# Row sums turned on TensorE, every unit of the probabilities split, values without zero columns: one change to an attention and MLP kernel

## What is computed

```python
q_rot, k_rot = (rotate(q), rotate(k))
scores = scale * np.matmul(q_rot, k_rot.transpose(0, 1, 3, 2))
scores = scores - np.max(scores, axis=-1, keepdims=True)
attn = np.exp(scores)
attn = attn / (np.sum(attn, axis=-1, keepdims=True) + 1e-09)
x = np.matmul(attn, v)                    # heads side by side: (4, 576, 512)
xk, xr = mu_k * x + (1 - mu_k) * x_prev, mu_r * x + (1 - mu_r) * x_prev
x = 1 / (1 + np.exp(-(xr @ w_r))) * (np.maximum(xk @ w_k, 0) ** 2 @ w_v)
u = x + (np.maximum(x.transpose(0, 2, 1) @ w_tok1, 0) @ w_tok2).transpose(0, 2, 1)
out = u + np.maximum(u @ w_ch1, 0) @ w_ch2
```

## Time and profile before

| | us |
|---|---|
| median of 3 runs (1092.89 to 1094.23) | 1093.23 |
| the profiled execution, device time | 1097.79 |
| its span, first to last instruction | 1095.7 |
| attention slots, from the first slot that weighs to the last | 26.4 to 433.8 |

### The profile page before, as it was taken

How to read it: one execution, slowest core, us unless ns; L and a number is a source line. 1 busy time by engine, 2 the same in 40 slices (tenths; PEclk the granted TensorE clock), 3 DMA queues, 4 the chain that set the end, 5 groups by cost and what they waited for, 6 DMA issues and landing times.

```text
span 1095.7 us, 21136 instructions
## 1 busy us (share of the span) xinstructions
PE 997.6 (91%) x6976; PEld 942.4 (86%) x6976; DVE 634.7 (58%) x1232; ACT 533.6 (49%) x1280; POOL 298.3 (27%) x291
## 2 busy tenths in 40 slices
PE   4977977787798797999999999999999999999997
PEld 4876866676687686999999999888999999999997
DVE  5977876786788797886778766456312212212220
ACT  4976866676787687454444434353211211221220
POOL 6656555555476654300000000135000000000000
PEclk9988988988989999999999999999999999999999
DMA  4223322222322221300000000031000000000000
GB/s 97 59 57 71 71 60 49 58 55 61 69 54 50 44 37 24 97 14 0 0 0 0 0 0 0 1 115 58 1 22 1 22 22 0 22 22 0 22 22 22
DMA packets 93629, 37.70 MB, mean 34 GB/s; under 512 B 84000, under 2 KB 84896, under 8 KB 93600
## 3 DMA queue, kind: packets, MB, share of 16 engines
q1 hardware_dynamic: 93312, 37.00, 14.8%
q10 hardware_dynamic: 288, 0.33, 0.1%
HBM read 32.51 MB, written 4.80 MB: 34 GB/s over the span
## 4 chain that ended last, share of the span: by engine, by line
PE 57%; DMA 22%; SPq 8%; issue 7%; DVE 3%; ACT 2%; POOL 1%; POOLq 0%; DVEq 0%; ACTq 0%
DMA sum_rows<-rsums 19%; PE psum L635 18%; PE psum L637 18%; PE psum L636 18%; SPq L363 3%; SPq L362 3%; SPq L384 1%; DMA raw_qk<-in_k_dram 1%; DMA raw_v<-in_v_dram 1%; PE psum L723 1%; PE psum L799 1%; PE psum L588 1%; DVE k_lo L1173 1%; ACT stage_out L998 0%; SPq L368 0%
## 5 line engine op out<-in xcount | busy, mean ns | idle before, releaser
L588 PE MATMUL psum<-kT_hi,qT 128*128 128x288 f32 x320 | 113.9, 369 | 53.6 <-ACT probs L837 48.9
L1003 ACT ACTIVATE h_hi<-psum 128x288 fp32r<-128x288 f32 x96 | 39.4, 410 | 245.9 <-PE psum L637 245.9
L606 PE MATMUL psum<-ident,probs 128*128 128x128 f32 x800 | 131.5, 292 | 8.1 <-DVE pT_lo L1071 3.8
L1054 DVE TENSOR_REDUCE neg_max<-psum 128x1 f32<-128x576 f32 (+1 forms) x160 | 120.5, 753 | 6.5 <-PE psum L588 4.0
L606 PEld LDWEIGHTS psum<-ident,probs 128*128 128x128 f32 x800 | 99.0, 149 | 28.2 <-DVE pT_lo L1071 17.6
L588 PEld LDWEIGHTS psum<-kT_hi,qT 128*128 128x128 f32 x320 | 67.2, 210 | 63.9 <-ACT probs L837 49.4
L837 ACT ACTIVATE probs<-psum,neg_max 128x576 f32<-128x576 f32 (+1 forms) x160 | 118.4, 740 | 5.8 <-DVE neg_max L1054 3.3
L1245 DVE SCALAR_TENSOR_TENSOR h_lo<-psum,h_hi 128x288 fp32r<-128x288 f32 x96 | 43.9, 458 | 125.8 <-ACT h_hi L1003 125.8
L635 PE MATMUL psum<-u_hi,wc_hi 128*128 128x288 f32 x384 | 114.2, 297 | 0.2 <-DVEq L1239 0.2
L635 PE MATMUL psum<-h_hi,wc_hi 128*128 128x288 f32 x384 | 113.7, 296 | 0.0
L636 PE MATMUL psum<-u_lo,wc_hi 128*128 128x288 f32 x384 | 113.3, 295 | 0.0
(11 more groups left out here) (127 smaller groups left out, 2786.0 us busy)
## 6 DMA issues: line engine op xcount, KB each, us to landing
stage_w<-in_moe_w_ch_dram SPq DMA_DIRECT2D x8, 768.0 KB, 4.4
rb<-sum_rows SPq DMA_DIRECT2D x32, 144.0 KB, 4.4
out_dram<-stage_out SPq DMA_DIRECT2D x8, 576.0 KB, 3.7
raw_qk<-in_q_dram SPq DMA_DIRECT2D x32, 128.0 KB
raw_qk<-in_k_dram SPq DMA_DIRECT2D x32, 128.0 KB
raw_v<-in_v_dram SPq DMA_DIRECT2D x32, 128.0 KB
w_raw<-in_moe_w_k_dram SPq DMA_DIRECT2D x4, 512.0 KB, 5.9
w_raw<-in_moe_w_v_dram SPq DMA_DIRECT2D x4, 512.0 KB, 5.6
```

The source lines that it names most:

```text
L588: ins = t.matmul(bank[:, x, 0:HALF], qT[i][:, tile * P:(tile + 1) * P], keys[:, x * HALF:(x + 1) * HALF], start=(n == 0), stop=(n == 1))
L606: ins = t.transpose(bank[:, at:at + P], probs[i][:, tile, at_key:at_key + P], ident[:, :])
L1003: a.activation(h2_hi[:, f, :], psum[:, f % 4, 0:HALF], ACT.Relu).then_inc(h2_hi_ready, 1)
L1054: d_.tensor_reduce(neg_max[0:m, at:at + 1], score_banks[at][0:m, :, 0:HALF], AX.XY, ALU.max, negate=True).then_inc(maxed, 1)
```

## The change

- `WHOLE` is empty. Unit 0 is split as the others are: DVE gets L0 (128x512), and V0 becomes four matmuls on `v_pair`. `raw_v` loses its zero columns.
- The exponents' sums go into columns 64 to 68 of a 128x128 tile, one tile for each head of a pair. After unit 2 of the first span PE transposes that tile behind the 256 columns of `o_bank`; ACT's copy O0 becomes 448 wide and brings the turned sums along; DVE inverts rows of 128 on 5 partitions; SP stores them as five rows of 512 bytes.
- `invert` moves from the start of DVE's slot to its end, behind M4 and ahead of O1, and now waits for O0 of ACT.
- The store and the read of the sums move in SP's list. For the even head the read comes a store and several loads later. For the odd one store and read stand together.
- The three orders change; the last slot's too.
- `k2_hi` and `k2_lo` begin lower, over the end of `stage_w`, so SP waits for the end of `gated` before it loads the channel weights.

```diff
-    WHOLE = (0,)
+    WHOLE = ()
...
-    ORDER = steps("T0 T1 S0 P0 S1 T2 V0 T3 V1 V2 T4 S2 T5 P1 S3 V3 T6 T7 S4 V4 V5 V6 V7")
-    ACT_ORDER = steps("H0 H1 P0 P1 P2 H2 E0 H3 v0 O0 E1 H4 H5 E2 H6 H7 P3 E3 O1 E4")
-    DVE_ORDER = steps("I0 M0 L1 P0 P1 L2 M1 L3 P2 O0 M2 L4 L5 M3 L6 L7 M4 P3 O1")
+    ORDER = steps("S0 T0 T1 P0 S1 T2 V0 T3 V1 T4 S2 V2 T5 P1 S3 T6 V3 V5 T7 V4 S4 V6 V7")
+    ACT_ORDER = steps("H0 H1 E0 P0 H2 P1 P2 H3 E1 v0 H4 O0 H5 P3 E2 H6 H7 E3 O1 E4")
+    DVE_ORDER = steps("M0 L0 L1 M1 L2 P0 P1 L3 P2 M2 L4 O0 L5 M3 P3 L6 L7 M4 I0 O1")
...
-    LAST_DVE_ORDER = steps("I0 L0 L1 X0 L2 X1 L3 O0 X2 L4 X3 L5 X4 L6 X5 L7 X6 O1 X7")
+    LAST_DVE_ORDER = steps("L0 L1 X0 L2 X1 L3 O0 I0 X2 L4 X3 L5 X4 L6 X5 L7 X6 O1 X7")
...
-        raw_v = [r(f"raw_v{i}", [P, NT, P]) for i in range(2)]
-        o_lo = r("o_lo", [P, SPAN[1][2]])
+        raw_v = [r(f"raw_v{i}", [P, NT, D]) for i in range(2)]
+
+        SUMS = SPAN[1][2]
+        o_lo = r("o_lo", [P, SUMS + P])
...
-        sums = r("sums", [P, 2, NT])
-        rsums = r("rsums", [P, 2, NT])
+        sums = r("sums", [P, 2, P])
+        inverted = r("inverted", [P, P])
...
-        r = Region(STAGE_END, RB)
+        r = Region(STAGE_END - (STAGE - KT * S) * FLOAT, RB)
...
-                sp.dma_start(sum_rows[bass.ds(it * 2 + kk, 1), :].rearrange("o (t p) -> p (o t)", p=P),
-                             rsums[:, kk % 2, :], allow_slow_non_contiguous=True).then_inc(sums_stored, 16)
+                at = kk % 2 * D
+                sp.dma_start(sum_rows[bass.ds(it * 2 + kk, 1), :].rearrange("o (t p) -> t (o p)", p=P),
+                             inverted[at:at + NT, :]).then_inc(sums_stored, 16)
...
                 if not start:
-                    sums_out(it, -1)
+                    sums_back(it, -2)
                     next_v(it, 0)
-                    sums_back(it, -1)
...
-                sums_out(it, 0)
+                if not start:
+                    sums_out(it, -1)
+                    sums_back(it, -1)
                 next_v(it, 1)
-                sums_back(it, 0, first=start)
                 if more:
                     next_qk(it, 1)
+                sums_out(it, 0)
...
+            sp.wait_ge(v_ready, KD * CHUNKS)
             with sp.Fori(0, B) as b:
...
-                if n == WHOLE[-1]:
+                if n == 0:
                     ins.then_inc(v_used, 1)
+                if keys[-1] == FULL and s == 0:
+                    pe.wait_ge(expd, upto(it, kk, NT, NT))
+                    ins = t.transpose(o_bank[:, SUMS:SUMS + P], sums[:, i, :], ident[:, :])
...
-                             accum_out=sums[0:m, i, tile:tile + 1]).then_inc(expd, 1)
+                             accum_out=sums[0:m, i, D + tile:D + tile + 1]).then_inc(expd, 1)
...
-                width = SPAN[s][2]
+                width = SUMS + P if s == 0 else SPAN[s][2]
...
-                dve.wait_ge(expd, upto(it, kk, NT, NT))
+                me = slice(i * D, i * D + NT)
+                dve.wait_ge(o_lo_ready, upto(it, kk, 2, 1))
...
-                d_.tensor_scalar(rsums[:, i, :], sums[:, i, :], 1e-9, None, ALU.add).then_inc(sum_plus, 1)
+                d_.tensor_scalar(inverted[me, :], o_lo[me, SUMS:SUMS + P], 1e-9, None, ALU.add).then_inc(sum_plus, 1)
```

More of the change, by code:

```diff
@@ L163, in attention_rwkv_mixer @@
         sin = r("sin", [P, NT, D])
-        RB = (END - S * FLOAT - 160) // 32 * 32
+        RB = (END - S * FLOAT - 32 - 3 * P * FLOAT) // 32 * 32
         assert r.at - base <= RB
@@ L382, in sums_back @@
                 if i == 0 and not first:
-                    sp.wait_ge(x_scaled, it)
+                    sp.wait_ge(x_scaled, it + (kk // 2 + 1))
                 sp.dma_start(rb[i * D:i * D + D, :], sum_rows[bass.ds(it * 2 + kk, 1), 0:S].to_broadcast([D, S])).then_inc(rb_in, 16)
@@ L432, in _ @@
             last = HEADS // 2 - 1
+            sums_back(last, -2)
+            next_v(last, 0)
             sums_out(last, -1)
-            next_v(last, 0)
             sums_back(last, -1)
[L436 to L439, removed]
+            for kk in range(2):
+                sums_out(last, kk)
+                sums_back(last, kk)
             sp.wait_ge(span_out, 2 * HEADS)
@@ L510, in _ @@
             pool.sem_inc(k_roped, 1)
+            pool.sem_inc(x_scaled, 1)
             pool.wait_ge(tables_in, 32)
@@ L888, in slot @@
                             act.wait_ge(omu_ready, 1)
-                            act.wait_ge(x_scaled, KD)
+                            act.wait_ge(x_scaled, KD + 1)
                         mix2(0, 0, n, after=False)
@@ L933, in gated @@
                 if more:
-                    act.wait_ge(x_scaled, HEADS // 2)
+                    act.wait_ge(x_scaled, HEADS // 2 + 1)
                     for m in range(2 * KD):
@@ L1073, in invert @@
             def invert(it, i, kk, first):
-                dve.wait_ge(expd, upto(it, kk, NT, NT))
+                me = slice(i * D, i * D + NT)
+                dve.wait_ge(o_lo_ready, upto(it, kk, 2, 1))
                 if not first:
                     dve.wait_ge(sums_stored, it * 32 + (16 * kk - 16))
-                d_.tensor_scalar(rsums[:, i, :], sums[:, i, :], 1e-9, None, ALU.add).then_inc(sum_plus, 1)
+                d_.tensor_scalar(inverted[me, :], o_lo[me, SUMS:SUMS + P], 1e-9, None, ALU.add).then_inc(sum_plus, 1)
                 dve.wait_ge(sum_plus, upto(it, kk, 1, 1))
-                d_.reciprocal(rsums[:, i, :], rsums[:, i, :]).then_inc(sum_inv, 1)
+                d_.reciprocal(inverted[me, :], inverted[me, :]).then_inc(sum_inv, 1)
             def write_x(it, i, kk, s):
@@ L1114, in slot @@
                             wait_for_room(dve)
-                            dve.wait_ge(x_scaled, KD)
+                            dve.wait_ge(x_scaled, KD + 1)
                         mix(0, 0, n)
@@ L1129, in _ @@
             d_.memset(sums[:, :, :], 1.0)
+            d_.memset(o_bank[:, SPAN[0][2]:SUMS], 0.0)
             for i in range(2):
@@ L1133, in _ @@
                     d_.memset(raw_qk[i][TAIL:P, j, FULL, :], 0.0)
-                d_.memset(raw_v[i][:, :, D:P], 0.0)
                 d_.memset(rot_q[i][:, NT, :], 0.0)
@@ L1180, in gated @@
                 if more:
-                    dve.wait_ge(x_scaled, HEADS // 2)
+                    dve.wait_ge(x_scaled, HEADS // 2 + 1)
                     for m in range(2 * KD):
```

## The result

| | before | changed |
|---|---|---|
| median, range | 1093.73 us (1092.89 to 1098.25, 4 runs) | 1042.68 us (1041.23 to 1043.5, 4 runs) |
| profiled execution, span | 1097.79, 1095.7 us | 1042.09, 1040.3 us |

The ratio is 0.9524, 95% interval 0.9495 to 0.9553: 51 us less. The forecast was 1059 us, 34 us less, and its range began at 1045 us. Direction and cause are as forecast; the size is that of rival 2, and the time lies outside the range.

What follows compares the result with a forecast made beforehand. SP's queue round, waiting for the store of the inverted sums, was taken as the bound. 31 slots at 13.14 - 11.99 us give 35.7, less 1.5 for the last slot: 1093.2 - 34.2 = 1059 us, range 1045 to 1078 us.

Steps and rivals of the forecast that it cites:

- rival 2: DVE's additions smaller than priced: slot 11.2 to 11.6 us, bounded by ACT and PE too, 1041 us at 11.4; chance 0.12.
- The store: Store of the inverted sums as 5 rows of 512 bytes: 3 us taken, between 2.3 and 9 to 12 us.
- The slot of 11.99 us: DVE's attention slot: undisturbed 10.45 us, less 0.20 wait, plus L0 0.68, reciprocal 0.77, addition 0.04 and 0.25.
- rival 1: Price is kept but the new order stalls DVE by 0.2 to 0.9 us a slot: 1065 to 1087 us; chance 0.20.
- The addition behind POOL's work: DVE's addition before the reciprocal waits for a POOL operation at a shared port: 0.25 us added, ends 0 and 1.06.
- PE, ACT and POOL at nothing: In attention slots, work on PE (10.9 us), ACT (9.95) and POOL (7.8) lies under DVE's 12 us: priced at nothing.
- The orders at nothing beyond their operands: In the slot's new orders, DVE's operands are ready before DVE in every step, by 0.3 us where tightest.
- Last slot 1.5 us: L0 and the longer inversion precede the mixing PE waits for: 1.5 us lost, between 0 and 1.9.
- Channel weights at nothing: Loads issued after PE's last matmul of `gated` land at about 703 and 707 us: nothing, or up to 1 us.
- The clock: PE's granted clock, 0.50 after long waits in disturbed slots, stays at 1.00 in the changed kernel.
- rival 3: Store stays at 9 to 12 us, POOL's split of v makes V0 late by 3.1 us every second slot: 1107 us; chance 0.05.
- rival 4: Short store doesn't free SP's queue, the read still waits ahead of loads: slot about 13, 1090 us; chance 0.04.

Runs made afterwards that it cites:

- the slow store: Changed kernel with each head's inverted sums stored once more as 640 single elements, the read and DVE's next inversion waiting for both stores: 1061.74 us.

## Why the prediction was right in kind and wrong in size

**What bounds the kernel: right.** The queue's round was the bound. Moving the read in SP's list gives 38 us; putting 5 to 6 us of store back costs 20.

**The store: right, but smaller than the lower end.** I took 3 us and had 2.3 as the lower end, from a load; SP could issue the read 1.25 us after it began with the store, and its longest wait is 1.3. The rule of the Trainium skill, page "DMA: Bandwidth & Descriptors", section "Rules for kernel authors", on a strided last dimension agrees with what the runs showed. The profile's page counts 93312 packets in the queue of SP's loads and stores before and 72640 after, 646 fewer for each of 32 stores, and 93280 with the slow store. 640 single elements took 5.4 to 6.4 us in one form and 9 to 12 in the other, and five rows no more than SP's 0.3 us of issuing and 1.3 us of waiting.

**DVE takes its place: right.** 97% busy, and doubled work of DVE shows in full.

**The slot of 11.99 us: wrong, it is 11.38.** The failed step is where I started from 10.45 us "since it holds the small gaps between instructions too" and added durations to it. The durations came out nearly as priced: the reciprocal 0.94 us for 0.96, L0 0.68, the addition 0.37 for about 0.46, and DVE's durations in a slot sum to 11.95 us. But I took the spacing of the old order as fixed. Added up from the rows of the two slots (a row of two instructions as one), 10.39 us of durations and a wait of 0.20 stood in the slot of 10.45, and 11.90 us of durations stand in the one of 11.40: the overlap of neighbours, less the gaps, grew from 0.14 to 0.50 us. That is 0.36 of the 0.59 us by which 11.99 misses this slot. The other 0.23 are durations, 1.51 us more where I had priced 1.74: 0.14 in the three additions and 0.09 in the steps that I held for unchanged. The profiled execution was forecast at 1063.6 us and took 1042.1; of these 21.5 us the slots are 20.5 (31 times 11.99 less 11.33). The median was missed by 16 only, since the profiled execution before stood 4.6 us above its median and the one after 0.6 below. I treated the orders only as a danger (rival 1, chance 0.20), never as a gain, so the range had no room below.

**The addition behind POOL's work: right, priced 0.08 us too dear.** It takes 207 to 452 ns here and stayed on DVE's path. It took 366 ns in one order and 598 in another, and in both it ended 0.07 to 0.12 us behind POOL's instruction. The rule of the Trainium skill, page "SBUF — State Buffer", section "Who interferes with whom", that the two engines take turns at a port agrees with that.

**PE, ACT and POOL at nothing: right at this slot.** But the cover is thin: 0.42 us more of ACT with three more transposes on PE costs 0.25 us.

**The orders at nothing beyond their operands: half right.** DVE waits for nothing, as I had followed it. What I had not followed is that the old lists with the new work would have cost 22 us more.

**Last slot 1.5 us: right,** 1.8 measured. **Channel weights at nothing: right.** SP issued them at 645.0 us and ACT took the first one up without a wait (a row with one would show it in brackets):

```profile
652.37 2.84 ACT L970 ACTIVATE wc_hi<-stage_w 128x1536 f32 x2
```

**The clock:** back at 1.00 in the slots, as forecast; outside the steady slots it is lower, 0.92 in the first slot (24 to 32 us) and 0.80 in the last (384 to 392 us), where PE had been busy for 3.1 of the 8 us before.

**Rivals.** Rival 1: no stall; DVE's wait list is empty. Rival 2: its slot of 11.4 us and its 1041 us came, but mostly for another reason: of the 0.59 us only 0.14 lie in smaller additions, and 0.36 in neighbours that stood closer. Rivals 3 and 4 didn't happen; in the slow-store run it is rival 4's round that decides, with rival 3's path close beside.

## What to carry to other kernels

When a queue's wait bounds a kernel, first move the waiting instruction behind the loads that don't need it: here that gave 38 of 40 us before any new code. Where the change then fills one engine, charge each new operation to that engine by start-to-start times, let the order of instructions count as a term that can go either way, and look for the same result in a cheaper shape: inverting 128x5 before the turn instead of 5x128 after it saved 20 us more, together with the addition of 1e-9, which that kernel leaves out. Lists of several engines are changed together: two of the ways to change only a part cost 62 and 116 us here.

## What the runs showed of the hardware that I had not expected

- DVE's instructions either overlap in the trace by 0.06 to 0.09 us or stand 0.02 to 0.04 apart, with nothing in between (changed kernel, 100 to 300 us). It goes with the half of the partitions that an instruction works on. L2 and L7, `pT_hi` of 64 partitions, read the upper half and stand apart from both neighbours in every slot there. O0 reads `o_lo` and writes `xT` on the half that belongs to its head, which changes from slot to slot, and its spacing changes with it: in the slot shown above it overlaps with its neighbours (304.04), and in the next it stands apart:

```profile
314.79 0.48 DVE L1080 TENSOR_TENSOR pT_lo<-psum,pT_hi 128x320 fp32r<-128x320 f32 x1
315.30 0.42 DVE L1098 TENSOR_TENSOR xT<-psum,o_lo 64x256 f32 x1
315.75 0.49 DVE L1080 TENSOR_TENSOR pT_lo<-psum,pT_hi 128x320 fp32r<-128x320 f32 x1
```

  An order was worth 0.42 us a slot by closer succession. No run changed the halves alone, so this is read from the rows and not tested.
- A store of 640 single elements took 9 to 12 us out of 128 partitions, with loads issued behind it and without, and 5.4 to 6.4 out of 5; what makes the difference stays open. It slows loads that run beside it: 512 KB landed in 3.5 to 3.6 us without it, in 3.2 to 3.8 where nothing was issued until it had landed, in 5.6 to 5.9 in the kernel before and in 9.4 to 10.2 where loads ran fully beside it.
- The kernel before, which waits for DMAs, differed by 1.1% between two chips; the changed one, with a full engine, by 0.1%.
